# One more round in TensorE's repeated body, the last state update dropped, and three waits moved, in a linear attention, Fourier and MLP kernel

## The reference, cut to what matters

```python
for t in range(S):                                   # _attn_ref
    y[:, :, t] = np.einsum('bhd,bhde->bhe', rt, state)
    Sa = np.einsum('bhde,bhe->bhd', state, at)
    state_decay = state * wt[:, :, None, :] - np.einsum('bhd,bhe->bhde', Sa, bt)
    state = state_decay + np.einsum('bhd,bhe->bhde', vt, kt)
...
X = np.fft.fft(np.fft.fft(x, axis=1), axis=2)        # _moe_ref
u = x + np.real(X)
un = (u - mean) / np.sqrt(var + 1e-06)
x = u + np.maximum(un @ w_ch1, 0.0) @ w_ch2
...
u = x + token_mlp(x)                                 # _moe2_ref
out = u + np.maximum(u @ w_ch1, 0.0) @ w_ch2
```

## Time and profile before

| | us |
|---|---|
| median of 3 runs | 995.66 |
| lowest, highest | 990.18, 1000.15 |
| the profiled execution | 994.72 |
| its span, first to last instruction | 992.6 |
| TensorE busy | 953.8 (96%) |
| VectorE (DVE), ScalarE (ACT), GpSimd (POOL) busy | 499.6, 349.1, 300.6 |

### The profile page before, as it was taken

The page is one execution under the profiler, slowest core; times in us unless marked ns, Lnnn a source line. Parts: engine busy times, 40 slices in busy tenths (PEclk is TensorE's granted clock), DMA queues, the critical chain, the costliest instruction groups (busy, mean ns, idle before and its releaser), DMA issues.

```text
span 992.6 us, 48525 instructions
## 1 busy us (share of the span) xinstructions
PE 953.8 (96%) x21454; PEld 909.3 (92%) x21454; DVE 499.6 (50%) x941; ACT 349.1 (35%) x758; POOL 300.6 (30%) x361
## 2 busy tenths in 40 slices
PE   6899999999999769999999999999999999999998
PEld 3788888889888769899999999999999999999998
DVE  4367767667676348766433334444843233223322
ACT  3465656566656424333211112232332122112211
POOL 6365565565655336905200000025600000000000
PEclk9899999999999889999999999999999999999999
DMA  8266666667665336401200000001100000000000
GB/s 254 97 186 195 195 197 202 194 217 245 212 204 168 113 102 186 127 22 49 78 1 0 0 0 0 0 0 53 41 1 21 20 0 20 20 20 7 13 20 20
DMA packets 50518, 86.80 MB, mean 87 GB/s; under 512 B 6336, under 2 KB 30016, under 8 KB 50464
## 3 DMA queue, kind: packets, MB, share of 16 engines
q1 hardware_dynamic: 48848, 81.96, 26.3%
q0 software_dynamic: 880, 3.69, 1.2%
q10 hardware_dynamic: 736, 0.48, 0.2%
HBM read 70.37 MB, written 7.86 MB: 79 GB/s over the span
## 4 chain that ended last, share of the span: by engine, by line
PE 92%; issue 3%; POOL 3%; DVE 1%; DMA 0%; ACT 0%; POOLq 0%; SPq 0%; DVEq 0%; ACTq 0%
PE d_bank L1538 13%; PE d_bank L1552 13%; PE pp L476 12%; PE c_bank L1538 11%; PE c_bank L1552 11%; PE pr L476 9%; PE ps L476 4%; PE f_bank L1247 3%; PE f_bank L1217 3%; POOL at L259 3%; PE t_bank L1687 2%; PE t_bank L1674 2%; PE ps L672 2%; PE ps L532 1%; PE pr L498 1%
## 5 line engine op out<-in xcount | busy, mean ns | idle before, releaser
L1454 ACT ACTIVATE d_h_hi<-d_bank 128x384 fp32r<-128x384 f32 x96 | 47.1, 491 | 197.3 <-PE d_bank L1538 197.3
L1491 DVE SCALAR_TENSOR_TENSOR d_h_lo<-d_bank,d_h_hi 128x384 fp32r<-128x384 f32 x96 | 53.6, 558 | 75.2 <-ACT d_h_hi L1454 75.2
L1552 PE MATMUL d_bank<-w_lo,d_h_hi 128*128 128x320 f32 x288 | 89.1, 309 | 0.0
L1552 PE MATMUL d_bank<-w_hi,d_h_hi 128*128 128x320 f32 x288 | 89.1, 309 | 0.0
L1552 PE MATMUL d_bank<-w_hi,d_h_lo 128*128 128x320 f32 x288 | 89.1, 309 | 0.0
L1454 ACT ACTIVATE c_h_hi<-c_bank 128x384 fp32r<-128x384 f32 x80 | 37.4, 489 | 143.3 <-PE c_bank L1538 143.3
L1552 PE MATMUL c_bank<-w_hi,c_h_hi 128*128 128x320 f32 x240 | 74.9, 312 | 0.0
L1552 PE MATMUL c_bank<-w_hi,c_h_lo 128*128 128x320 f32 x240 | 74.3, 309 | 0.0
L1552 PE MATMUL c_bank<-w_lo,c_h_hi 128*128 128x320 f32 x240 | 74.2, 309 | 0.0
L1503 DVE TENSOR_TENSOR d_o<-d_bank,u_all 128x320 f32<-128x320 f32 x24 | 11.8, 492 | 111.0 <-PE d_bank L1552 111.0
L1491 DVE SCALAR_TENSOR_TENSOR c_h_lo<-c_bank,c_h_hi 128x384 fp32r<-128x384 f32 x80 | 42.2, 554 | 37.4 <-ACT c_h_hi L1454 37.4
(11 more groups left out here) (271 smaller groups left out, 2787.7 us busy)
## 6 DMA issues: line engine op xcount, KB each, us to landing
e_raw<-in_e SPq DMA_DIRECT2D x72, 256.0 KB, 4.3
r_raw<-in_c SPq DMA_DIRECT2D x24, 768.0 KB, 4.3
tok<-tok_of SPq DMA_DIRECT2D x24, 320.0 KB, 2.7
e_raw<-in_e SPq DMA_DIRECT2D x24, 260.5 KB, 4.0
va<-in_c SPq DMA_DIRECT2D x24, 160.0 KB, 2.5
vb<-in_c SPq DMA_DIRECT2D x24, 160.0 KB, 2.7
attention_out<-yout SPq DMA_DIRECT2D x92, 40.0 KB, 2.0
stage<-in_moe_w_ch POOLq DMA_DIRECT2D x4, 640.0 KB, 5.7
```

Of the source, the lines that this page charges most:

```text
L1454: nc.scalar.activation(h_hi[:, m, :], bank[m % 4][:, 0:TW], ACT.Relu).then_inc(h_hi_done, 1)
L1491: nc.vector.scalar_tensor_tensor(h_lo[:, m, :], bank[m % 4][:, 0:TW], 0.0, h_hi[:, m, :].bitcast(F32), ALU.max, ALU.subtract).then_inc(h_l ...
L1552: last = nc.tensor.matmul(bank[4 + t % 2][:, 0:E], lhs, rhs, start=(m == 0 and i == 0), stop=(m == NM - 1 and i == 2))
```

## The change

Five edits:

1. TensorE's repeated body runs rounds 1 to 24, and only rounds 25 and 26 stand written out. The body's round 24 also runs `tokk` for a group 24 that does not exist: four transposes of what `kt` holds.
2. `upd_k`, `upd_b`, `xt` and the load `vb` are left out for group 23.
3. In `first_pieces` the wait for `y_done` moves from the start to just before bank 2 (n = 2).
4. The three rests for the MLP c are made behind `diff 2`, ahead of `p 2` and `q 2`.
5. The first values of the MLP's three counters come from TensorE, ahead of its wait for the weights, and not from DVE. This holds for both MLPs.

```diff
+STATE_ONLY = ("upd_k", "upd_b", "xt", "vb")
...
-                if 0 <= g + ahead < NG:
+                if 0 <= g + ahead < (NG - 1 if name in STATE_ONLY else NG):
                     run(name, g + ahead)
...
-        with pe.Fori(FIRST, NG):
+        with pe.Fori(FIRST, NG + 1):
             for name, ahead in ORDER_PE:
                 unit(name)
-        for g in range(NG, NG - min(a for _, a in ORDER_PE)):
+        for g in range(NG + 1, NG - min(a for _, a in ORDER_PE)):
             for name, ahead in ORDER_PE:
-                if g + ahead < NG:
+                if g + ahead < (NG - 1 if name in STATE_ONLY else NG):
                     unit(name, g + ahead)
...
-                    if b == B - 1 and (name, t) == ("q", HT - 1):
+                    if b == B - 1 and (name, t) == ("diff", HT - 1):
                         for f in range(3):
                             start.rest(dve, f, bank[START_BANKS[f]])
...
             def first_pieces():
-                pe.wait_ge(y_done, NG)
                 pe.wait_ge(early.tok_lo_done, HT)
                 pe.wait_ge(lo_done, N1)
                 pe.wait_ge(added, NA)
...
                         f0, m = KF[f]
+                        if n == 2:
+                            pe.wait_ge(y_done, NG)
                         for i in tiles:
...
-            dve.sem_inc(t_lo, 3)
-            dve.sem_inc(h_lo_done, NM)
-            dve.sem_inc(y_done, TB)
             loop(dve, pre, main)
...
+            pe.sem_inc(t_lo, 3)
+            pe.sem_inc(h_lo_done, NM)
+            pe.sem_inc(y_done, TB)
             ahead.weights_split(pe)
             loop(pe, pre, main)
```

## The result

| | before | changed |
|---|---|---|
| median of 20 runs, us | 995.91 | 989.44 |
| lowest, highest | 990.18, 1000.58 | 987.98, 993.30 |
| profiled execution, span | 994.72, 992.6 | 990.62, 988.4 |

The ratio is 0.9931, with a 95% interval from 0.9917 to 0.9945: 6.9 us less (5.5 to 8.3); the two medians differ by 6.5. Differences in us that stand beside a ratio are worked out from the ratio. The forecast was 987.0 and 8 us less, within a range from 982.5 to 992.0.

The account below looks back on a forecast made before the run. TensorE was taken to bound the kernel, idling in written out rounds for blocks of code. Gains of 7.6 (up to the Fourier part) - 0.1 (MLP c) + 0.45 (MLP d) = 7.95 us gave 986.8, forecast 987.0, range 982.5 to 992.

Parts of the forecast that it names:

- Straight code is fetched in blocks: Written out rounds: next block asked for on entering the present one, takes 4.1 us; a block at full speed lasts 2.1.
- 350.0 + 4.1 = 354.1: Round 25, `upd_b`: second block usable at 354.1, needed at about 352.0, so a stop of 2.1 us.
- 4.1 us each: Round 24 before: two blocks of code between 335.15 and 343.35, read as 4.1 us each.
- The sum for edit 1: Round 24 in the body: 6.88 - 1.1 + 0.2 = 6.0 us earlier at `y` of group 22.
- The 0.4 for the missing load `vb`: End of attention: without `vb` behind it in SP's queue, `cp` lands 0.4 us sooner, at most 2.1.
- I gave it 0.2 us: Start of the Fourier part: clock at 0.50 for the first 0.4 us loses 0.2, so 7.8 becomes 7.6.
- rival (d): Fourier part: clock stays at 0.50; 16 us of it eat up the gain, 24 us give 999; chance 0.04.
- The MLP starts: MLP c: -0.1 us, gain at m = 0 given back at m = 1; MLP d: 0.45 us gained.
- The sum: Whole kernel: 7.6 - 0.1 + 0.45 = 7.95 us less, a time of 986.8, forecast 987.0.
- Rival (a): Behind the body: first block asked for at the body's end, not on entering matmul 102; 985.3 us; chance 0.20.
- (b): Body's end: the block behind it isn't there, one stop of 4.1 us; 991.1 us; chance 0.10.
- (c): Rounds 24 and 25: another engine or a load paces them, attention's end doesn't move; 993 to 995 us; chance 0.04.

Follow-up runs that it names:

- the run without edit 3: The changed kernel with the wait for `y_done` back at the start of `first_pieces`: 989.38 us, ratio 0.9924 to the kernel before.
- the second profile of the changed kernel: The changed kernel timed and profiled once more, nothing altered, on another chip: 989.68 us, ratio 0.9918 to the kernel before.
- edit 1 alone: The kernel before with only TensorE's repeated body running round 24 too: 993.03 against 996.38 us, ratio 0.9956.
- edit 2 alone: The kernel before with only `upd_k`, `upd_b`, `xt` and the load `vb` left out for group 23: 996.33 against 996.38 us, ratio 0.9994.

## Why the prediction was right, and where it was off

**Straight code is fetched in blocks.** Right, and this is what bears the gain. `m3` of group 23 was forecast at 342.13 and came at 342.11; five or six fewer packets on q8 were six; in the run with one round more written out that round took 6.6 us more. The page of the Trainium skill that speaks for unrolling (Runtime: NRT & Kernel Launch, Instruction fetch mechanics) gives the wrong sign for this engine and this code: in the traces the body's branch cost at most 0.35 us, put down to POOL, and behind the body's new end TensorE waited 0.79 us for ACT, with no stop for code.

**Round 25.** The places were right, `sol2` and `upd_b`, and the first block came at 350.07, forecast 350.0. The stop before it was 0.78 us and not 1.8, because TensorE came to it later: its clock was low (mean 0.55) from 345.5 to 349.1, which the sum didn't have. The step that failed in the profile is "350.0 + 4.1 = 354.1": the second block took 5.70 us and came at 355.77. The trace of before had a sign of this that the prediction averaged away. Its two blocks of "4.1 us each" are 3.78 and 4.42, and the longer one began with these rows:

```profile
338.93 0.30 PE L476 MATMUL pp<-tok,rv_t 64*64 64x40 f32 x2 [1.66 <-issue]
```

```profile
339.32 0.33 SPq L194 DMA_DIRECT2D r_raw<-in_c  x1
```

It is the load of r, 0.4 us behind the request. The edit moves the block limits against the loads: TensorE now asks for the second block 0.7 us behind the issue of 768 KB. Without that collision it was 354.14 (the run without edit 3). `y` of group 22, forecast 13.4 us behind `m3`, was 14.9 in this profile and 12.9 to 13.7 in four others of the same tail, so over these the term was near. The sum for edit 1 has a slip as well: it adds the 0.2 us that the longer stops cover and leaves out the 0.2 that the clock costs. And ACT's work in round 24 was a little more than in the round before, 7.98 against 7.75 us, which held nothing up.

**Edits 2 and 3.** The last `y` was forecast at 363.25 and came at 363.71, which is luck in part: `y` of group 22 came 1.5 us too late, and the way from it to the last `y` was 6.72 us and not 7.75, with `cp` landing after 3.1 us and `y_k` and `y_b` at full clock. The 0.4 for the missing load `vb` isn't shown: `cp` landed after 2.8 to 4.2 us in the four profiles with it and after 2.5 to 4.0 in the ten without. That DVE's counters behind tile 2's load would take over from `y` was right (L1185). The size was off: tile 2 took 4.0 us and not 2.3, so 366.46 instead of 363.8. In the second profile of the changed kernel the same counter held TensorE for 1.5 us, in that without edit 3 for none. That edit 3 brings nothing that can be told is shown by its removal. What stretched the load isn't shown; a block's packet, SP's and POOL's stores ran beside it.

**The clock at the Fourier part.** Over both profiles the term that was mis-sized most: I gave it 0.2 us. The stretch from the first Fourier matmul to the turn went from 77.28 to 78.73 and 80.83 in the two profiles of the changed kernel, so 1.5 to 3.6, of which the clock is some 1.5 and 3. My rival (d) had the mechanism, but with 16 us of low clock where there were 3 to 6, and I took 0.2 because the row of before showed full clock there. That row was one execution. There the low stretch, behind the wait of 2.09 us for `cp`, fell on `y_k`, `y_b` and the 64 matmuls of the update and was over before the Fourier part; edit 2 takes the 64 away. That this alone moves the low clock into the Fourier part is my reading and not shown: with edit 1 alone the 64 are there and it moved as well.

**The MLP starts.** Right in mechanism and size: +0.15 for c (forecast +0.1), -0.40 for d (-0.45), both together not measurable.

**The sum.** 7.95 forecast, 6.9 measured over 20 runs, 4.1 between the two profiles. That the time came within the range owes something to errors that offset each other in part: the dearer second block, the slow tile and the clock against the quicker way to the last `y`. The profile of before had a full clock at the Fourier part, and that of the changed kernel both the collision and the slow tile. Rival (a) is out by its own sign: the first stop was 0.76 to 2.15 us in all ten profiles of this tail and ended 6.4 to 7.8 us behind the body's end, where (a) had 5.9; from matmul 102 it is 3.1 to 4.5. (b) is out by the row at 343.22, and (c) by the window of round 24.

## What to carry to other kernels

Where an engine issues small instructions fast, count its blocks of code: idle time that is put down to "issue" at regular distances, with a packet on its instruction queue in each, is the price of straight code. Running one more pass of the repeated body, even with a unit that does nothing useful, was cheaper here than writing the pass out. Then look which chain the next block limit cuts: 64 needless matmuls ahead of a link of that chain cost 4 us. An edit that brings nothing alone can bring 3 us behind another, so try it on both. And ask behind which wait a counter's first value stands, and what the clock will be where work starts earlier; both took back part of what the profile of before promised.

## What the hardware showed that I had not expected

- A large load issued 0.7 us ahead of a block's request delayed the block from 3.8 to between 5.4 and 5.7 us; issued 1.8 us ahead it hardly did.
- The clock behind an idle TensorE can cost more than the wait: the way to the turn took 77.3 to 78.7 us with full clock at its start and 78.7 to 81.2 with 2 to 6 us of 0.50. With six matmuls on constants in a wait of some 2 us, and the early load, the clock stayed at 1.00.
- Leaving work out can bring nothing: with edit 2 alone 64 matmuls, an addition and a load less gave no time that could be told, and the same edit behind edit 1 gave some 3 us.
